# The upper part of SBUF of a fused attention and mixer kernel begins 224 bytes lower

## The chip, the cores and the metric

The kernel runs on one core of one Trainium2 chip. The metric is the device time of one execution in microseconds. All matrix products are float32-accurate: most operands are split into a high and a low part (type fp32r) and three products are added.

## The reference

Attention over 4 batches of 12 heads (sequence 448, head size 64, capped scores) gives x of (4, 448, 768). Two mixer layers follow:

```python
scores = cap * np.tanh(scale * q @ k.T / cap)         # scale = 1/8
x = softmax(scores) @ v                               # heads side by side: (4, 448, 768)

theta = x @ w_theta                                   # 768 x 768
y = w_tok_r @ (x * cos(theta)) + w_tok_i @ (x * sin(theta))   # 448 x 448 each, over tokens
u = x + y
x = u + relu(u @ w_ch)                                # 768 x 768

h = relu(x.T @ w_tok1) @ w_tok2                       # 448 -> 256 -> 448, over tokens
u = x + h.T
out = u + relu(u @ w_ch1) @ w_ch2                     # 768 -> 1536 -> 768, the MLP
```

## The kernel before, in words

**Stages.** TensorE works through five stages, each written out as a fixed order of instructions with semaphore waits. The times are those of the profiled execution.

- Attention, to about 179 us: 24 pairs of heads. `score` makes scores 448 columns wide with two 64-row matmuls side by side, `weigh_slot` and `sum_keys` multiply by values and by ones.
- Angles and token mixing, 179 to 388 us, by batch: `angles(b)` multiplies x (x_hi, x_lo as weights) by theta (moving, 384 columns), and `mix_tokens(b, half)` multiplies z (weights) by the token matrices (moving, 448 columns).
- Channel and token layers, 388 to 551 us, by batch: `channel(b, e)` has channel_hi, channel_lo as weights and u as the moving operand, 448 columns, in sets of 18 matmuls. `turn` transposes. `tokens_up` has tok1 as weights and 384 columns moving, in sets of 24. `tokens_down` has hidden as weights and tok2 as the moving operand, 448 columns, six matmuls for each feature tile; three of those in a row are 18 matmuls.
- MLP, 547 us to the end: four blocks of tokens k = 0 to 3 (512, 384, 512, 384 wide). For each of the twelve weight tiles c, `up(k, c)` does 18 matmuls with wide as the moving operand and `down(k, c)` does 18 with relu. The order is up 0, up 1, down 0, up 2, down 1, and so on to up 11, down 10, down 11. Every one of them reads its weights from tile mlp[c] and moves 512 or 384 columns.

`products` (L1047 to L1051) issues the three matmuls of one split product: hi by hi (L1049), hi by lo (L1050), lo by hi (L1051). In the program matmul(out, weights, moving), the trace prints the moving operand and the weights of a matmul in no fixed order.

**Placement.** SBUF addresses are written out by hand, as byte offsets within a partition. BASE is 16512 = 64.5 x 256. The constants lie from there; x_t begins at 17664 = 69 x 256; the working memory AT_WORK (L63) at 60672 = 237 x 256, and the upper memory AT_TOP (L64) at 167392 = 653 x 256 + 224. Every tensor in the working and the upper memory lies a multiple of 256 bytes behind the start of its region. In the working memory are x_hi and x_lo, z, u, wide, rows, hidden, and the MLP's tiles 0, 1 and 7 to 10, with one relu buffer; tile 11 and two relu buffers lie in the second half of x_t. In the upper memory lie, one after another in time:

- theta_hi, theta_lo, token_hi, token_lo (L142 to L145), moving operands;
- channel_hi, channel_lo and their raw copy (L187 to L190), tok1_hi, tok1_lo (L191, L192), weights, and tok2_hi, tok2_lo (L193, L194), moving operands;
- the MLP's tiles 2 to 6, weights, by

```python
tile_at = ([AT_EARLY + 12288 * j for j in range(2)] + [AT_TOP + 12288 * j for j in range(5)]
           + [AT_ROWS + 12288 * j for j in range(4)] + [AT_X + X_BYTES // 2])
```

Within a tile, one matmul's weights are 128 elements of 4 bytes, at multiples of 512 bytes.

**Other engines.** The DMA queue of SyncE loads raw weights into place (L482, L485 for the MLP's tiles, as soon as the memory is free). GpSimd (`split`, L537 to L542), ScalarE (L755) and VectorE (L1027) split them into hi and lo in place. ScalarE and VectorE also take results out of PSUM.

Of the kernel before, what the change touches and what calls it, by code (L numbers as in the profile page):

```python
# [58 lines left out]
BASE = 16512  # L59
# [1 line left out]
AT_X = AT_SMALL + 1152  # L61
X_BYTES = BATCH * D_TILES * SEQ * 4
AT_WORK = AT_X + X_BYTES  # L63
AT_TOP = BASE + 150848 + 32  # L64


def mixer_kernel(nc, kq_t, v, cap, w_theta, w_tok_r_t, w_tok_i_t, w_ch, w_tok1, w_tok2,
                 w_ch1, w_ch2, out_t, sum_scratch, inverse_scratch, u_scratch):
    ctx = ExitStack()
    with ctx:  # L70
        def place(name, shape, dtype, offset):
            return nc.alloc_sbuf_tensor_at(name, shape, dtype, offset=offset)
# [65 lines left out]
        o += 2 * SUM_F * 4  # L138
        assert o <= AT_TOP


        theta_hi = place("theta_hi", [P, D_TILES, MODEL], F32R, AT_TOP)  # L142
        theta_lo = place("theta_lo", [P, D_TILES, MODEL], F32R, AT_TOP + 18432)
        token_hi = place("token_hi", [P, MIX_TILES, SEQ], F32R, AT_TOP + 36864)
        token_lo = place("token_lo", [P, MIX_TILES, SEQ], F32R, AT_TOP + 49408)  # L145
        o = AT_WORK
# [36 lines left out]
        turns = [turns0, place("turns1", [P, HALF], F32, o)]  # L183
        assert o + 1536 <= AT_TOP

# [1187 lines left out]
```

## Time and profile before

| what | value |
| --- | --- |
| median of 3 runs | 907.78 us (905.97 to 907.85) |
| profiled execution | 907.67 us |
| its span, first to last instruction | 905.6 us |
| TensorE busy, matmuls | 888.3 us, 5248 instructions |
| VectorE, ScalarE, GpSimd busy | 438.0, 305.4, 189.0 us |
| mean granted TensorE clock | 0.995 |

The page gives busy time and counts; the timeline gives each instruction with its start. In the timeline a matmul's duration includes its way through the array, so successive matmuls overlap: the distance from start to start, called the pitch here, is what a matmul costs. A pitch over a long run is the difference between two starts, divided by the number of matmuls between them, which the loops give.

### The profile page before, as it was taken

The page shows a single profiled execution, that of the slowest core. Times are in us where ns is not written, and L with a number is a line of the kernel's source. Part 1 is how long each engine was busy: PE and PEld are TensorE (multiplying, and loading weights), DVE is VectorE, ACT ScalarE, POOL GpSimd, SP SyncE. Part 2 cuts the span into 40 slices and gives each one's busy share as a digit, 9 for nine tenths or more (in the row PEclk, how much of TensorE's full clock was granted, in tenths as well). Part 3 has the DMA queues.
Part 4 walks back from the last instruction along what each step waited for, and adds up shares of the span by engine and source line. Part 5 has one row for each costly group of instructions (what it writes and reads, how often), then busy time and mean ns, then how long its engine had stood idle before and what let it go on. Part 6 is the DMA issues. An engine that isn't in the chain of part 4 may idle for free.

```text
span 905.6 us, 12431 instructions
## 1 busy us (share of the span) xinstructions
PE 888.3 (98%) x5248; PEld 746.3 (82%) x5248; DVE 438.0 (48%) x593; ACT 305.4 (34%) x355; POOL 189.0 (21%) x139
## 2 busy tenths in 40 slices
PE   8999999998999999999999999999999999999998
PEld 5455544498999889999999998888899988889998
DVE  5799988889484976824342433311400130003002
ACT  6989997644151433502121221111100100001000
POOL 0345535147050442451000005800000000000000
PEclk9999999999999999999999999999999999999999
DMA  7555674412020100330000115500220030002001
GB/s 175 160 133 146 176 175 115 124 43 62 1 70 1 39 23 1 106 111 1 1 0 1 62 47 187 176 1 1 70 71 1 1 105 0 1 1 71 1 1 53
DMA packets 42119, 56.84 MB, mean 63 GB/s; under 512 B 7344, under 2 KB 37456, under 8 KB 42064
## 3 DMA queue, kind: packets, MB, share of 16 engines
q1 hardware_dynamic: 41840, 55.82, 21.3%
q8 instruction: 42, 0.69, 0.3%
q10 hardware_dynamic: 224, 0.23, 0.1%
q14 instruction: 13, 0.11, 0.0%
HBM read 41.62 MB, written 8.52 MB: 55 GB/s over the span
## 4 chain that ended last, share of the span: by engine, by line
PE 88%; DVE 7%; issue 2%; ACT 1%; DMA 0%; POOL 0%; DVEq 0%; ACTq 0%
PE psum L1049 23%; PE psum L1050 23%; PE psum L1051 23%; PE psum L1091 8%; PE psum L1061 5%; PE psum L1066 2%; PE psum L1118 2%; DVE sin_z L899 1%; PE psum L1214 1%; DVE reduced L892 1%; DVE reduced L888 1%; DVE wide_lo L936 1%; ACT wide_hi L697 1%; PE psum L1164 1%; DMA kq_raw<-kq_t 0%
## 5 line engine op out<-in xcount | busy, mean ns | idle before, releaser
L1032 DVE SCALAR_TENSOR_TENSOR relu_lo<-psum,relu_hi 128x512 fp32r<-128x512 f32 (+1 forms) x48 | 30.0, 624 | 275.1 <-ACT relu_hi L761 217.3
L761 ACT ACTIVATE relu_hi<-psum 128x512 fp32r<-128x512 f32 (+1 forms) x48 | 26.2, 545 | 307.8 <-PE psum L1051 298.1
L1049 PE MATMUL psum<-wide_hi,mlp 128*128 128x512 f32 (+1 forms) x288 | 105.0, 365 | 0.4 <-DVE wide_lo L936 0.4
L1051 PE MATMUL psum<-wide_hi,mlp 128*128 128x512 f32 (+1 forms) x288 | 104.9, 364 | 0.0
L1051 PE MATMUL psum<-relu_hi,mlp 128*128 128x512 f32 (+1 forms) x288 | 104.8, 364 | 0.0
L1049 PE MATMUL psum<-relu_hi,mlp 128*128 128x512 f32 (+1 forms) x288 | 104.8, 364 | 0.0
L1050 PE MATMUL psum<-wide_lo,mlp 128*128 128x512 f32 (+1 forms) x288 | 104.8, 364 | 0.0
L1050 PE MATMUL psum<-relu_lo,mlp 128*128 128x512 f32 (+1 forms) x288 | 104.7, 364 | 0.0
L1091 PE MATMUL psum<-ring,values 128*32 128x448 f32 x768 | 81.4, 542 | 1.4 <-issue 1.2
L633 ACT ACTIVATE ring<-psum,score_scale 128x1792 f32<-128x1792 f32 (+1 forms) x48 | 75.2, 1566 | 18.8 <-PE psum L1118 10.3
L636 ACT ACTIVATE ring<-ring,cap_col 128x1792 f32<-128x1792 f32 (+1 forms) x48 | 77.1, 1606 | 1.6
L1049 PEld LDWEIGHTS psum<-wide_hi,mlp 128*128 128x128 f32 x288 | 54.0, 188 | 7.0 <-DVE wide_lo L936 1.1
L1091 PEld LDWEIGHTS psum<-ring,values 128*32 128x32 f32 x768 | 23.0, 109 | 44.5 <-issue 44.2
L1050 PEld LDWEIGHTS psum<-relu_lo,mlp 128*128 128x128 f32 x288 | 54.1, 188 | 6.1
L1051 PEld LDWEIGHTS psum<-wide_hi,mlp 128*128 128x128 f32 x288 | 54.0, 188 | 6.1
L1051 PEld LDWEIGHTS psum<-relu_hi,mlp 128*128 128x128 f32 x288 | 54.1, 188 | 6.1
L1050 PEld LDWEIGHTS psum<-wide_lo,mlp 128*128 128x128 f32 x288 | 54.0, 188 | 6.1
L1049 PEld LDWEIGHTS psum<-relu_hi,mlp 128*128 128x128 f32 x288 | 54.0, 188 | 6.0
L1049 PE MATMUL psum<-theta_hi,x_hi 128*128 128x384 f32 x168 | 58.7, 349 | 0.0
L1050 PE MATMUL psum<-theta_lo,x_hi 128*128 128x384 f32 x168 | 56.5, 336 | 0.0
L1051 PE MATMUL psum<-theta_hi,x_lo 128*128 128x384 f32 x168 | 56.5, 336 | 0.0
L1049 PE MATMUL psum<-u_hi,channel_hi 128*128 128x448 f32 x144 | 54.1, 375 | 0.0
(135 smaller groups left out, 1977.2 us busy)
## 6 DMA issues: line engine op xcount, KB each, us to landing
kq_raw<-kq_t SPq DMA_DIRECT2D x47, 224.0 KB, 3.8
mlp_raw<-moe_w_ch SPq DMA_DIRECT2D x24, 384.0 KB, 6.8
values<-v SPq DMA_DIRECT2D x48, 112.0 KB, 3.3
inverse_rows<-inverse_scratch SPq DMA_DIRECT2D x12, 448.0 KB, 6.0
x_batch<-x_t SPq DMA_DIRECT2D x4, 1344.0 KB, 6.4
u_scratch<-x_t SPq DMA_DIRECT2D x2, 1344.0 KB, 5.6
out_t<-x_t SPq DMA_DIRECT2D x4, 672.0 KB, 3.4
theta_raw<-moe_w_theta SPq DMA_DIRECT2D x6, 384.0 KB, 4.5
```

The source lines that it names most:

```text
L633: act.activation(places, psum[:, first:end, 0:SEQ], ACT.Tanh, scale=score_scale[:, :]).then_inc(tanh_done, 1)
L636: act.activation(places, places, ACT.Exp, scale=cap_col[:, :]).then_inc(probs_ready, 1)
L697: act.activation(wide_hi[:, :, 0:BLOCKS[k][1] - BLOCKS[k][0]], x_block(k), ACT.Copy).then_inc(u_hi_made, 1)
L761: act.activation(relu_hi[c % 3][:, 0:n_tokens], psum[:, c % 2, 0:n_tokens], ACT.Relu).then_inc(relu_hi_made, 1)
L1032: dve.scalar_tensor_tensor(out=relu_lo[c % 3][:, 0:n_tokens], in0=psum[:, c % 2, 0:n_tokens], scalar=0.0, in1=relu_hi[c % 3][:, 0:n_tokens ...
L1049: pe.matmul(out, left[0], right[0], start=start, stop=False)
L1050: pe.matmul(out, left[0], right[1], start=False, stop=False)
L1051: return pe.matmul(out, left[1], right[0], start=False, stop=stop)
L1061: b_mm = pe.matmul(psum[:, b_tile, 0:SEQ], left[s][b_rows, b_keys], right[s][b_rows, queries], start=step == 0, stop=step == 2 and b_tile ...
L1066: a_mm = pe.matmul(psum[:, a_tile, 0:SEQ], left[s][a_rows, a_keys], right[s][a_rows, queries], start=step == 0 and a_tile != T, stop=step ...
L1091: mm = pe.matmul(psum[rows, VALUES_BANK, 0:SEQ], own[:, block, 32 * h:32 * h + 32], ring[:, ring_place(pair, tile), :], start=n == 0, stop ...
L1118: mm = pe.matmul(psum[32 * n:32 * n + 32, SUMS_BANK, 0:SEQ], weights[:, :], moving, start=True, stop=True)
```

## The change

One constant is changed. The upper memory begins at BASE + 150656 = 167168 = 653 x 256, where it began at BASE + 150880 = 167392. Everything placed relative to AT_TOP moves down by 224 bytes. The last tensor below it (sums) ends at 167104. No instruction, wait or size changes.

```diff
--- before.py
+++ after.py
@@ -61,7 +61,7 @@
 AT_X = AT_SMALL + 1152
 X_BYTES = BATCH * D_TILES * SEQ * 4
 AT_WORK = AT_X + X_BYTES
-AT_TOP = BASE + 150848 + 32
+AT_TOP = BASE + 150656
 
 
 def mixer_kernel(nc, kq_t, v, cap, w_theta, w_tok_r_t, w_tok_i_t, w_ch, w_tok1, w_tok2,
```

## Rows read from the trace of the kernel before

**Rows 1.** The page: busy time by engine; shares of the chain that ended last.
```profile
PE 888.3 (98%) x5248; PEld 746.3 (82%) x5248; DVE 438.0 (48%) x593; ACT 305.4 (34%) x355; POOL 189.0 (21%) x139
...
PE 88%; DVE 7%; issue 2%; ACT 1%; DMA 0%; POOL 0%; DVEq 0%; ACTq 0%
```
**Rows 2.** Stretches: length, busy PE, PEld, DVE, ACT, POOL, clock, DMA share, GB/s.
```profile
213.00:262.00 49.00, 49.00 (x263) 46.43 (x262) 35.41 (x56) 17.52 (x34) 16.61 (x14) 0.99 0.11 32
...
300.00:330.00 30.00, 27.77 (x151) 25.94 (x150) 28.77 (x45) 14.84 (x31) 15.60 (x14) 1.00 0.16 47
...
392.00:548.00 156.00, 155.95 (x831) 144.83 (x830) 63.09 (x88) 31.90 (x44) 21.80 (x14) 1.00 0.11 37
548.00:650.00 102.00, 102.00 (x448) 83.64 (x447) 27.36 (x33) 16.54 (x24) 26.43 (x19) 1.00 0.21 68
```
**Rows 3.** TensorE's waits, the longest: us in total, times, longest us.
```profile
PE psum L1049 <- DVE sin_z L899: 4.8, 2, 2.5
```
**Rows 4.** Timeline of TensorE, MLP block 0: start us, length us, instruction.
```profile
571.95 0.39 PE L1049 MATMUL psum<-wide_hi,mlp 128*128 128x512 f32 x1
...
605.54 0.39 PE L1049 MATMUL psum<-wide_hi,mlp 128*128 128x512 f32 x1
...
622.02 0.39 PE L1049 MATMUL psum<-wide_hi,mlp 128*128 128x512 f32 x1
...
646.50 0.39 PE L1049 MATMUL psum<-relu_hi,mlp 128*128 128x512 f32 x1
```
**Rows 5.** The same view, MLP block 1.
```profile
666.27 0.34 PE L1049 MATMUL psum<-wide_hi,mlp 128*128 128x384 f32 x1
...
691.71 0.33 PE L1049 MATMUL psum<-wide_hi,mlp 128*128 128x384 f32 x1
...
704.26 0.33 PE L1049 MATMUL psum<-wide_hi,mlp 128*128 128x384 f32 x1
...
722.98 0.33 PE L1049 MATMUL psum<-relu_hi,mlp 128*128 128x384 f32 x1
```
**Rows 6.** The same view: tokens_up, channel, tokens_down of batch 0.
```profile
421.02 0.34 PE L1049 MATMUL psum<-rows_hi,tok_hi 112*128 112x384 f32 x1
...
425.26 0.37 PE L1049 MATMUL psum<-u_hi,channel_hi 128*128 128x448 f32 x1
...
428.97 0.36 PE L1049 MATMUL psum<-tok_hi,hidden_hi 128*128 128x448 f32 x1
...
429.57 0.37 PE L1049 MATMUL psum<-tok_hi,hidden_hi 128*128 128x448 f32 x1
...
432.64 0.36 PE L1049 MATMUL psum<-u_hi,channel_hi 128*128 128x448 f32 x1
```
**Rows 7.** The same view: scores of pairs 8 and 9 of heads.
```profile
61.09 0.36 PE L1066 MATMUL psum<-kq_hi,kq_lo 64*128 64x448 f32 x1
...
62.33 0.36 PE L1066 MATMUL psum<-kq_hi,kq_lo 64*128 64x448 f32 x1
...
67.76 0.36 PE L1061 MATMUL psum<-kq_lo,kq_hi 64*128 64x448 f32 x1
...
69.18 0.36 PE L1061 MATMUL psum<-kq_hi,kq_lo 64*128 64x448 f32 x1
```
**Rows 8.** The same view: token mixing of batch 1, then angles of batch 2.
```profile
259.19 0.45 PE L1049 MATMUL psum<-token_hi,tail_hi 128*128 128x448 f32 x1
...
284.90 0.34 PE L1049 MATMUL psum<-theta_hi,x_hi 128*128 128x384 f32 x1
...
288.03 0.27 PE L1164 MATMUL psum<-ident,x_batch 128*128 128x128 f32 x1
```
**Rows 9.** Splits of the MLP's tiles, duration min/median/max in ns; timeline of GpSimd.
```profile
L539 POOL CAST mlp<-mlp_raw x14: 823/826/1435, 400.5 to 582.7; 128x768 fp32r<-128x768 f32 x14
...
L1027 DVE TENSOR_TENSOR mlp<-mlp_raw,mlp x10: 958/959/2345, 563.6 to 635.8; 128x768 fp32r<-128x768 f32 x10
...
543.29 0.82 POOL L539 CAST mlp<-mlp_raw 128x768 fp32r<-128x768 f32 x1 [131.60 <-DMA mlp_raw<-moe_w_ch]
```

## The prediction

> **What bounds the kernel now.** I read the page first: TensorE is busy 98% of the span and the chain that ended last is 88% TensorE [rows 1]. Then I read the table of stretches. It shows TensorE busy 49.00 of 49.00 us busy in the stretch of 213 to 262 us, 155.95 of 156.00 us in the channel and token stretch, and 102.00 of 102.00 us in the first MLP block, at a granted clock of 0.99 to 1.00, the upper of its two levels (2.4 GHz) [rows 2]. The table of TensorE's waits has nine rows and 13 us in all, none of it for a DMA; the longest is 4.8 us in two waits for the angles [rows 3]. A busy share of 100% doesn't say that the engine streams at its best pace, since a matmul's record (0.39 us) is longer than the distance between two starts (0.23 us). So the view that decides here is the timeline of TensorE, read as pitch: start of one matmul to the start of the next. Any pitch that shrinks moves the end almost one for one.
>
> **The natural experiment in the trace.** The MLP uses twelve weight tiles of one shape in one loop, up(c) and down(c-1) by turns, 18 matmuls each. Tiles 2 to 6 begin at AT_TOP + 12288 j. AT_TOP is 167392 = 653 x 256 + 224, which is 32 beyond a multiple of 64; all other tiles, and the moving operands wide and relu, begin on multiples of 256. For 512 columns, from the start of up(0,3) at 571.95 to that of up(0,7) at 605.54 lie eight phases, 144 matmuls, that all read tiles 2 to 6: 33.59 / 144 = 233.3 ns. From up(0,9) at 622.02 to down(0,11) at 646.50 lie six phases, 108 matmuls, of tiles 8 to 11: 24.48 / 108 = 226.7 ns [rows 4]. For 384 columns the same two stretches are 25.44 / 144 = 176.7 ns and 18.72 / 108 = 173.3 ns [rows 5]. Instruction, clock, moving operand and neighbours are the same; the place of the weights is what differs. So weights in the upper memory cost 6.6 ns per matmul of 512 columns and 3.4 ns per one of 384.
>
> **The change, part by part.** It adds and removes no instruction and no wait. It moves everything that is placed from AT_TOP down by 224 bytes, to 653 x 256.
>
> *MLP.* Five tiles x 36 matmuls x two blocks of 512 columns: 360 x 6.6 = 2.4 us. The two blocks of 384: 360 x 3.4 = 1.2 us. Together 3.6 us, all on the path.
>
> *tok1 weights.* 192 matmuls of 384 columns take their weights there. One set of 24 runs from 421.02 to 425.26: 176.7 ns [rows 6], the slow pace of 384. At the good one: 192 x 3.4 = 0.65 us.
>
> *Channel weights.* 432 matmuls of 448 columns. The set of 18 that follows runs from 425.26 to 428.97, 206.1 ns [rows 6]. No row shows an ordinary 448-column matmul of all 128 rows with both operands on a multiple of 64, so I bound it. Lower bound: the line through the two good paces, 173.3 at 384 and 226.7 at 512, gives 200.0 at 448, a gain of 432 x 6.1 = 2.6 us. Upper bound: the scores are 448 columns wide and have both operands on multiples of 256; pair 8 of heads runs at 1.24 us for six steps, 206.7 ns, so the gain may be 0. Pair 9 runs at 1.42 us for seven, 202.9 ns [rows 7]. The token mixing (weights low, moving operand high) has 25.71 / 126 = 204.0 ns with its first gap in it [rows 8], and a set of tok2 3.67 / 18 = 203.9 [rows 6]. Three of four rows lie near 203.3, so I take that: 432 x 2.8 = 1.2 us.
>
> *Upper memory as the moving operand.* theta (504 matmuls, 384 columns): from 284.90 to 288.03, 3.13 / 18 = 173.9 ns [rows 8], the good pace but for 0.6, so between nothing and 0.3 us is to be had; I take nothing. token and tok2 (648 matmuls, 448 columns): between 200.0 (a gain of 648 x 4 = 2.6 us) and the 206.7 of pair 8 (a loss of 1.8 us). theta says that a moving operand off the boundary costs nothing, and pair 9 that 203 is what 448 columns do on aligned operands, so I take 203.5 and 0.3 us.
>
> *Writers and transfers.* GpSimd, ScalarE and VectorE split weights in either memory. For the MLP's tiles, on and off the boundary mixed, the shortest and the middle duration are 823 and 826 ns on GpSimd, 958 and 959 on VectorE [rows 9]; the move is worth nothing to them. The loads into the upper memory may take a little less or more: GpSimd waits for the tiles' data, but TensorE waits for none of that [rows 3]. Tile 2's data are there at 543.29 [rows 9], and TensorE comes to it two phases of 4.2 us before the 571.95 of [rows 4], at about 563.6. With some 6 us for the split in between, a landing would have to slip by over 10 us to cost anything. Where the matmuls get faster, nothing else is late: in the MLP stretches VectorE is busy 27 of 102 us and ScalarE 17 [rows 2]. Only around the angles do the chains of VectorE and GpSimd set the pace (2.2 us idle in the stretch from 300 to 330, and the 4.8 us above) [rows 2, 3], and the move doesn't touch those.
>
> **A rule against it.** The Trainium skill, "SBUF — State Buffer", section Specifications (TRN2), gives SBUF 16-byte cachelines and names no wider grid for speed. Both 167392 and 167168 are multiples of 16, so by that rule the move does nothing and the time stays at 907.7 us, as in the fourth rival below. The rows disagree with it as the whole story: 233.3 against 226.7 ns between operands that all begin on multiples of 16. The same page, Operand start alignment, treats a start as a matter of legality and says it timed nothing.
>
> **The sum.** The profiled execution took 907.67 us (span 905.6, 2.05 around it), 0.1 under the median of 907.78. 3.6 + 0.65 + 1.2 + 0.3 = 5.75, so 907.7 - 5.8 = 901.9 us, 0.63% less.
>
> **The rivals.**
> First, everything goes to the floor: misplacement, of either operand, is all that 448 columns suffer from. Then 3.6 + 0.65 + 2.6 + 2.6 = 9.45, 898.3 us. For it: the first three matmuls of a tok2 set take 0.60 us, 200 ns each [rows 6]. Against: pairs 8 and 9, aligned and at 207 and 203; theta, off the boundary and free.
> Second, the 448-column streams keep what they have or fall into the slow rhythm of pair 8: only 4.25 us of the MLP and tok1 remain (903.4), or 4.25 - 1.8 = 2.45 us (905.2). For it: the channel's 206.1 is nearly pair 8's pace with everything aligned.
> Third, slower: what marks tiles 2 to 6 is that they lie high, not their residue, and the move brings moving operands onto the residue of their weights (x_hi and theta, z and token, hidden and tok2 differ by 224 now). If equal residues collide, 648 matmuls go from 204.0 to 206.7 (+1.8 us) and theta's 504 from 173.3 to 176.7 (+1.7): 911.2 us. It ends slower only if the MLP's and tok1's 4.25 us stay out, since they would outweigh its 3.5. Against: MLP tiles 7 to 11 share their residue with wide and relu and are the fast ones.
> Fourth, the change doesn't do what it says: the border is one of place. The highest fast tile ends at 158976 and the lowest slow one begins at 167392, so no row excludes a border between them. Then nothing moves, 907.7. Against: tok1's, channel's and the five tiles' weights, spread over 60 KB, all lose alike, while theta, in the same place, loses nothing as a moving operand.
>
> **How the numbers follow.** Forecast (901.0 to 903.0) 0.48; all to the floor 0.22; 448 columns unchanged or slow 0.17; place alone 0.09; slower 0.04. A measurement of this kernel can tell about 0.2% (1.8 us) from no change. Faster are the first three, 0.87; the same 0.09; slower 0.04. For 8 in 10 the range takes the forecast, the floor and the milder half of the third case (903.4 but not 905.2), with 0.8 us of scatter at the low end and 1.0 at the high one: 897.5 to 904.4.
>
> **What would show it.** In the profile of the changed kernel the eight phases from up(0,3) to up(0,7) should take 144 x 226.7 = 32.6 us in place of 33.6, and the 384-column ones 25.0 in place of 25.4; tok1's sets 4.16 in place of 4.24. The channel's 18 matmuls at 3.60 us speak for the floor, 3.66 for the forecast, 3.71 for the second rival; the token stretch of 126 at 25.2 us for the floor, 25.7 for the forecast. Stages before 179 us should not change. I am wrong if the upper tiles keep 233.3 ns, or if another operand, theta above all, takes up a pitch over 173.3.

## The result, and the profile after

The changed kernel takes 903.82 us (median of 13 runs, 900.37 to 906.29) against 907.85 us (13 runs, 905.45 to 910.65). The ratio is 0.9949, 95% interval 0.9933 to 0.9966: 4.6 us less (3.1 to 6.1), which is the distance of the two means; the medians are 4.0 apart. A good part of the scatter goes with the granted TensorE clock: of the changed kernel's 13 executions the one at a mean of 0.998 took 900.37 us and the one at 0.992 took 906.29. The forecast was 901.9 us and 5.8 us less, with a range of 897.5 to 904.4.

The profiled execution took 904.51 us, its span is 902.5. The page's line of busy times answers to [rows 1]; TensorE is still busy 98% of it.
```profile
PE 885.0 (98%) x5248; PEld 745.9 (83%) x5248; DVE 436.8 (48%) x593; ACT 305.7 (34%) x355; POOL 188.5 (21%) x139
```
The timeline of TensorE after, in the MLP's blocks 0 and 1 (start us, length us, instruction). From up(0,3) to up(0,7), and from up(1,3) to up(1,7), as in [rows 4, 5]:
```profile
572.45 0.39 PE L1049 MATMUL psum<-wide_hi,mlp 128*128 128x512 f32 x1
...
605.09 0.39 PE L1049 MATMUL psum<-wide_hi,mlp 128*128 128x512 f32 x1
...
665.60 0.33 PE L1049 MATMUL psum<-wide_hi,mlp 128*128 128x384 f32 x1
...
690.55 0.33 PE L1049 MATMUL psum<-wide_hi,mlp 128*128 128x384 f32 x1
```
32.64 / 144 = 226.7 ns where it was 233.3, and 24.95 / 144 = 173.3 where it was 176.7. All twelve tiles now have the good pace.

The 448-column stages after, same view: the channel's first two sets of batch 0, then a tok1 set and the channel set behind it (to answer to [rows 6]), then the token mixing of batches 1 and 3, whose ends are 285.45 and the 389.07 above (to answer to [rows 8]).
```profile
389.07 0.37 PE L1049 MATMUL psum<-u_hi,channel_hi 128*128 128x448 f32 x1
...
396.51 0.27 PE L1214 MATMUL psum<-ident,block_t 128*112 128x128 f32 x1
...
421.74 0.34 PE L1049 MATMUL psum<-rows_hi,tok_hi 112*128 112x384 f32 x1
...
425.93 0.36 PE L1049 MATMUL psum<-u_hi,channel_hi 128*128 128x448 f32 x1
...
429.58 0.36 PE L1049 MATMUL psum<-tok_hi,hidden_hi 128*128 128x448 f32 x1
```
```profile
259.83 0.45 PE L1049 MATMUL psum<-token_hi,tail_hi 128*128 128x448 f32 x1
...
285.45 0.34 PE L1049 MATMUL psum<-theta_hi,x_hi 128*128 128x384 f32 x1
...
362.96 0.45 PE L1049 MATMUL psum<-token_hi,tail_hi 128*128 128x448 f32 x1
```
The channel knows two rhythms: 7.44 / 36 = 206.7 ns in the first sets and 3.65 / 18 = 202.8 in most later ones (steady 206.7 in five of the 24 sets and 202.7 in nineteen; all 24 had 206.7 before). Token mixing has 25.62 / 126 = 203.3 in batch 1, but 26.11 / 126 = 207.2 in batch 3, which was 25.85 / 126 = 205.2 before:
```profile
362.39 0.45 PE L1049 MATMUL psum<-token_hi,tail_hi 128*128 128x448 f32 x1
...
388.24 0.36 PE L1049 MATMUL psum<-u_hi,channel_hi 128*128 128x448 f32 x1
```
A wait has grown. TensorE's waits for wide_lo (us in total, times, longest), first before, then after:
```profile
PE psum L1049 <- DVE wide_lo L936: 0.4, 1, 0.4
...
PE psum L1049 <- DVE wide_lo L936: 1.9, 2, 1.6
```
The timelines of GpSimd and VectorE there, first after, then before:
```profile
543.16 1.84 POOL L541 TENSOR_TENSOR mlp<-mlp_raw,mlp 128x768 fp32r<-128x768 f32 x1
...
543.42 4.79 DVE L936 TENSOR_TENSOR wide_lo<-x_t,wide_hi 128x3072 fp32r<-128x3072 f32 x1 [1.45 <-ACT wide_hi L697]
```
```profile
544.12 3.36 DVE L936 TENSOR_TENSOR wide_lo<-x_t,wide_hi 128x3072 fp32r<-128x3072 f32 x1 [1.44 <-ACT wide_hi L697]
...
544.20 4.97 POOL L541 TENSOR_TENSOR mlp<-mlp_raw,mlp 128x768 fp32r<-128x768 f32 x1
```
Before, VectorE began 0.08 us ahead of GpSimd: its subtraction took 3.36 us and GpSimd's took 4.97 in place of 1.84. After, tile 2's data had landed a little earlier, GpSimd began 0.26 us ahead, and VectorE's took 4.79. TensorE stood for 1.6 us before up(0,0), where it had stood 0.4; from the last tok1 matmul to up(0,0) it is 1.89 us in place of 0.39, 1.5 more.

Where the time went, by stage, from the starts on the timeline (us):

| stage | before | after |
| --- | --- | --- |
| attention, to the first theta matmul | 178.86 | 179.44 |
| angles and token mixing | 209.38 | 209.63 |
| channel and token layers, to the first MLP matmul | 159.29 | 159.20 |
| MLP, to the end | 358.10 | 354.24 |
| from the angles to the end | 726.77 | 723.07 |

The last row is the one to compare between single profiles: in the profiles of this study the attention stage ended anywhere from 175.79 to 182.25 us, although no kernel changes anything that TensorE, ScalarE or VectorE read there. Part of that is the clock: from 12 to 22 us the granted clock was 0.66 after and 1.00 before. By groups of matmuls (sums of pitches) the 3.7 us are: MLP -2.6 at 512 columns and -1.2 at 384, channel -1.1, tok1 -0.4, tok2 -0.2, theta -0.1, token +0.4, and the wait for wide_lo +1.5.

### The profile page after: what moved, and what is told of

Same layout as the page of the kernel before. It is cut to its first block, busy times and chain, and to the rows that moved or that the text cites. A ratio compares the mean times of both kernels' runs of the same rounds, so it can differ in the third digit from the quotient of the medians.

```text
span 902.5 us, 12431 instructions
## 1 busy us (share of the span) xinstructions
PE 885.0 (98%) x5248; PEld 745.9 (83%) x5248; DVE 436.8 (48%) x593; ACT 305.7 (34%) x355; POOL 188.5 (21%) x139
## 4 chain that ended last, share of the span: by engine, by line
PE 89%; DVE 6%; issue 2%; ACT 1%; POOL 0%; DVEq 0%; POOLq 0%; ACTq 0%
PE psum L1049 23%; PE psum L1051 23%; PE psum L1050 23%; PE psum L1091 9%; PE psum L1061 5%; PE psum L1066 3%; PE psum L1118 2%; DVE sin_z L899 1%; PE psum L1214 1%; DVE wide_lo L936 1%; DVE reduced L892 1%; DVE reduced L888 1%; PE psum L1124 1%; ACT wide_hi L697 1%; PE psum L1164 1%
## 5 line engine op out<-in xcount | busy, mean ns | idle before, releaser
L1049 PE MATMUL psum<-token_hi,z_hi 128*128 128x448 f32 x144 | 53.4, 371 | 0.5 <-POOL z_lo L592 0.5
```

What stands on the lines that cost most here:

```text
L1049: pe.matmul(out, left[0], right[0], start=start, stop=False)
```

## Experiments

The theory of the prediction was that weights must begin on a boundary. Its rivals were the place (high memory), and, new after the result, the distance between the start of the weights and that of the moving operand. "Distance" is weights minus moving operand, modulo 256.

**The lower tiles off the boundary, the upper ones on it.**
```diff
-        tile_at = ([AT_EARLY + 12288 * j for j in range(2)] + [AT_TOP + 12288 * j for j in range(5)]
-                   + [AT_ROWS + 12288 * j for j in range(4)] + [AT_X + X_BYTES // 2])
+        tile_at = ([AT_EARLY + 32 + 12288 * j for j in range(2)] + [AT_TOP + 12288 * j for j in range(5)]
+                   + [AT_ROWS + 32 + 12288 * j for j in range(4)] + [AT_X + X_BYTES // 2])
-        ring_at = [o, AT_X ...
+        ring_at = [o + 256, AT_X ...
```


> The changed kernel, but the MLP's six tiles in the lower memory (0, 1, 7 to 10) begin 32 bytes past a multiple of 256, and the five in the upper memory stay on it. Theory of the residue: every phase of tiles 0, 1, 7 to 10 takes the slow pace (233.3 ns a matmul at 512 columns, 176.7 at 384; 4.20 and 3.18 us a phase), tiles 2 to 6 and 11 the good one (226.7 and 173.4). That is 6 x 36 x 2 x (6.6 + 3.4) = 4.3 us more than the changed kernel, about 908. Rival of the place (what counts is that weights lie above 160 KB): all tiles keep the pace of the changed kernel, about 904.

One execution: 909.74 us (the kernel before, same chip, 908.51). Its timeline: up(0,3) to up(0,7) on upper tiles; up(0,9) to up(0,11), four phases on tiles 8 to 10; the same four at 384 columns.
```profile
575.05 0.39 PE L1049 MATMUL psum<-wide_hi,mlp 128*128 128x512 f32 x1
...
607.70 0.39 PE L1049 MATMUL psum<-wide_hi,mlp 128*128 128x512 f32 x1
...
624.38 0.40 PE L1049 MATMUL psum<-wide_hi,mlp 128*128 128x512 f32 x1
...
641.18 0.39 PE L1049 MATMUL psum<-wide_hi,mlp 128*128 128x512 f32 x1
...
706.68 0.34 PE L1049 MATMUL psum<-wide_hi,mlp 128*128 128x384 f32 x1
...
719.17 0.35 PE L1049 MATMUL psum<-wide_hi,mlp 128*128 128x384 f32 x1
```
Upper tiles 32.65 / 144 = 226.7 ns, lower ones 16.80 / 72 = 233.3. The roles have changed places, so the rival of the place falls. But at 384 columns the lower tiles have 12.49 / 72 = 173.5, not the expected 176.7: weights 32 beyond the boundary are free there, weights at 224 were not. The whole MLP stage takes 358.88 us, 4.6 more than the changed kernel's, which looks like the 4.3 of the theory but is chance: the six tiles cost 432 x 6.6 = 2.9 us at 512 columns and next to nothing at 384, and 1.65 us are in up(0,0) (5.85 us for 18 matmuls, 4.20 at 233.3 ns). There eight matmuls started 427 ns apart, at a granted clock of 0.50 from 550 to 553 us, the lower of the two levels (1.2 GHz), after TensorE had stood 1.8 us for wide_lo.

**A residue for each tile.** Tiles shifted by (160, 192, 0, 32, 64, 96, 224, 32, 64, 96, 128, 0) bytes, tok1 and tok2 moved on by 256 to make room.

> The changed kernel with each MLP tile at a residue of its own, modulo 256: tiles 0 to 11 at 160, 192, 0, 32, 64, 96, 224, 32, 64, 96, 128, 0. If a multiple of 64 is what weights need, tiles 1, 2, 4, 8, 10 and 11 have 226.7 ns and tiles 0, 3, 5, 6, 7, 9 (odd multiples of 32) have 233.3. If it is 256, as in the words of the change, only tiles 2 and 11 are fast; if it is 128, tiles 2, 10 and 11. The residue modulo 256 may also give more than two paces.

908.03 us in one execution. Two of its phases at 512 columns, up(0,1) (residue 192) and up(0,10) (residue 128):
```profile
554.02 0.39 PE L1051 MATMUL psum<-wide_hi,mlp 128*128 128x512 f32 x1
...
558.15 0.39 PE L1051 MATMUL psum<-relu_hi,mlp 128*128 128x512 f32 x1
...
629.30 0.39 PE L1051 MATMUL psum<-wide_hi,mlp 128*128 128x512 f32 x1
...
633.49 0.39 PE L1051 MATMUL psum<-relu_hi,mlp 128*128 128x512 f32 x1
```
4.13 and 4.19 us, against 4.08 at the good pace. The steady pitches (the second half of each phase, from the starts, ns; a range is over up and down and the tiles of that residue):

| residue | 0 | 32 | 64 | 96 | 128 | 160 | 192 | 224 |
| --- | --- | --- | --- | --- | --- | --- | --- | --- |
| 512 columns | 226.7 | 233.2-233.6 | 233.3-233.7 | 233.9-235.0 | 232.2-233.3 | 233.3 | 228.9 | 233.0-233.3 |
| 384 columns | 173.3 | 173.3 | 174.3-176.8 | 173.3-176.4 | 175.3-176.1 | 176.7-177.1 | 173.3 | 173.3-176.4 |

Multiples of 64 or 128 don't do. Of eight residues only 0 has the good pace at both widths. At 384 columns one residue can have either pace (224: 173.3 in up, 176.4 in down), so something besides the residue plays a part there, perhaps the tile read just before.

**The moving operands off, the weights on.** wide and relu, high and low, begin 32 bytes on; what lies behind wide moves by 256.
```diff
-        wide_hi = place("wide_hi", [P, D_TILES, BANK], F32R, o)
-        wide_lo = place("wide_lo", [P, D_TILES, BANK], F32R, o + 12288)
-        o += 24576
+        wide_hi = place("wide_hi", [P, D_TILES, BANK], F32R, o + 32)
+        wide_lo = place("wide_lo", [P, D_TILES, BANK], F32R, o + 12288 + 32)
+        o += 24576 + 256
```


> The changed kernel, all weights on multiples of 256, but the MLP's moving operands (wide and relu, high and low parts) begin 32 bytes past one. Theory (only the start of the weights counts, as theta seemed to say): pitches stay at 226.7 and 173.4 ns. Rival (the distance between the two starts counts): 233.3 and 176.7 everywhere, 1728 x 5 = 8.6 us more than the changed kernel.

912.34 us in one execution. The same four starts as at the top:
```profile
572.46 0.39 PE L1049 MATMUL psum<-wide_hi,mlp 128*128 128x512 f32 x1
...
606.06 0.39 PE L1049 MATMUL psum<-wide_hi,mlp 128*128 128x512 f32 x1
...
668.16 0.34 PE L1049 MATMUL psum<-wide_hi,mlp 128*128 128x384 f32 x1
...
693.60 0.34 PE L1049 MATMUL psum<-wide_hi,mlp 128*128 128x384 f32 x1
```
33.60 / 144 = 233.3 and 25.44 / 144 = 176.7 ns, with all weights on multiples of 256, and so in every tile but for the first phase. The MLP takes 362.68 us where the changed kernel takes 354.24: 8.4 more, 8.6 were the rival's. The theory that only the start of the weights counts is refuted. The distance is 0 - 32 = -32 here, and it was 224 - 0 = -32 in [rows 4, 5]: the same two pitches.

**Both off.** Every tensor from the channel on, weights and moving operands alike, 32 bytes on (AT_TOP + 32, AT_WORK + 32 for u and what follows, tile 11 and the relu buffers + 32).

> The changed kernel with weights and moving operands of all stages after the token mixing 32 bytes past a multiple of 256, so that both have one residue. Theory (the start of the weights by itself): 233.3 and 176.7 ns in all twelve MLP tiles, 8.6 us more than the changed kernel, and 206 to 207 in the channel. Rival (their distance): 226.7 and 173.4 everywhere.

898.80 us in one execution; 721.01 us from the angles to the end. Its timeline: up(0,3) to up(0,7); a theta set; the token mixing of batch 1.
```profile
566.75 0.39 PE L1049 MATMUL psum<-wide_hi,mlp 128*128 128x512 f32 x1
...
599.39 0.39 PE L1049 MATMUL psum<-wide_hi,mlp 128*128 128x512 f32 x1
```
```profile
235.23 0.34 PE L1049 MATMUL psum<-theta_hi,x_hi 128*128 128x384 f32 x1
...
238.41 0.27 PE L1164 MATMUL psum<-ident,x_batch 128*128 128x128 f32 x1
...
256.07 0.45 PE L1049 MATMUL psum<-token_hi,tail_hi 128*128 128x448 f32 x1
...
281.36 0.33 PE L1049 MATMUL psum<-theta_hi,x_hi 128*128 128x384 f32 x1
```
32.64 / 144 = 226.7 ns with not one operand of the MLP on a multiple of 64. It is the distance of the two starts, not either start. theta tests its sign: its distance, x_hi minus theta, was 0 - 224 = +32 before and is 0 - 32 = -32 here. This set has 3.18 / 18 = 176.7 ns, the pace of distance -32 at 384 columns, which 11 of this run's 28 theta sets have; the other 17 have a steady 173.4. And the token stretch has 25.29 / 126 = 200.7 with its first gap in it, a steady 200.0, the floor that the prediction had worked out (e9 comes back to it).

**Distance 256.** The upper tiles, tok1 and tok2 are 256 bytes further on, on even multiples of 256, with the moving operands on odd ones.

> The changed kernel with the MLP's upper tiles (2 to 6) and tok1, tok2 256 bytes further on, so that they lie on even multiples of 256 while the moving operands stay on odd ones. If a distance of a multiple of 256 is what counts, tiles 2 to 6 keep 226.7 and 173.4 ns and the channel its 202.7 to 206.7. If it must be a multiple of 512, tiles 2 to 6 have more (229 to 233 ns at 512 columns).

904.72 us in one execution.
```profile
572.69 0.39 PE L1049 MATMUL psum<-wide_hi,mlp 128*128 128x512 f32 x1
...
605.33 0.39 PE L1049 MATMUL psum<-wide_hi,mlp 128*128 128x512 f32 x1
```
32.64 / 144 = 226.7: a distance of 256 is as good as 0. The grid of 256 bytes is right, for the distance.

**One part of the change: the weights alone.** theta, token and tok2 keep residue 224 (their offsets + 224), channel, tok1 and the tiles are as changed.

> One part of the change: channel, tok1 and the MLP's upper tiles are on a multiple of 256 as in the changed kernel, while theta, token and tok2, which are moving operands, keep residue 224. By my sum of the change this holds 5.45 of its 5.75 us, the rest being token and tok2. From the trace of the changed kernel I now expect slightly more: the token stretches had 204.0 to 204.5 ns before and 202.9 or 206.7 after, 0.4 us more in all, so this kernel should be level with the changed one within 0.5 us, and its token stretches at the pitches of before.

903.84 us (12 runs), ratio to the kernel before 0.9961 (0.9944 to 0.9977). From the angles to the end it takes 722.81 us against 723.07, and its token stretches have the steady pitches of before (203.3 in batch 1, 204.4 in batch 3). The gain of the change is that of the weights, as forecast.

**GpSimd waits for wide_lo.** In the loop over the MLP's tiles, on the changed kernel, and on the kernel before:
```diff
             for c in range(C_TILES):
+                if c == 2:
+                    pool.wait_ge(u_lo_made, BATCH + 1)
                 pool.wait_ge(mlp_loaded[c], 32)
```


> The changed kernel, and GpSimd waits for wide_lo of block 0 before it splits the MLP's tile 2. Theory: in the changed kernel's trace VectorE's wide_lo took 4.79 us where it took 3.36 before, because GpSimd's subtraction began 0.26 us ahead of it and held it up; TensorE stood 1.6 us before up(0,0). With the wait wide_lo takes 3.3 to 3.4 us, TensorE's wait for it falls to about 0.4 us, and the time falls by 1.2 us against the changed kernel (about 902.6). Rival (wide_lo's length is from something else, or TensorE is held by ScalarE's wide_hi): no change.

902.45 us (6 runs), ratio to the kernel before 0.9947 (0.9930 to 0.9964), where the changed kernel's is 0.9949: the times don't separate the two. The trace does (VectorE's and GpSimd's timelines, TensorE's wait; the two added lines shift the line numbers by 2):
```profile
544.58 3.36 DVE L938 TENSOR_TENSOR wide_lo<-x_t,wide_hi 128x3072 fp32r<-128x3072 f32 x1 [1.44 <-ACT wide_hi L699]
```
```profile
PE psum L1051 <- DVE wide_lo L938: 0.4, 1, 0.4
```
The channel and token stage takes 157.45 us against 159.20. So the collision is real. It costs 1.4 us (0.46 us from the last tok1 matmul to up(0,0), in place of 1.89) where 1.2 were expected. The other 0.3 of the 1.75 are not its doing: none of the channel's 24 sets has the slow rhythm here, and five had it in the changed kernel. Elsewhere this execution was slower: 26.12 us for batch 1's token mixing, the slow rhythm, in place of 25.62, and 27.66 for batch 2's in place of 26.64, with a granted clock of 0.72 from 316 to 322 us where the changed kernel had 1.00 (315 to 321). So from the angles to the end there is only 0.5 us between them. What follows matters for every reading at 448 columns: the two kernels give TensorE the same instructions and addresses, and yet batch 1's tokens run at a steady 202.7 ns in one profile and at 206.7 in the other.

> The kernel before with the same wait of GpSimd as in the run before. In its profiled execution wide_lo had won the race (3.36 us, TensorE waited 0.4 us). If it always wins there, no change (within 0.3 us); if the race goes either way from one execution to the next, up to 0.6 us faster on the median.

907.73 us (12 runs), ratio 1.0011 (0.9999 to 1.0023): no gain, and the stage takes 159.29 us, to the hundredth what it took without the wait. The race, without the wait, in the profiles: won by VectorE before and in e2, e3 and e4, lost after and in e1, e5, e7 and e10. In these profiles VectorE began wide_lo 5.39 to 5.40 us after the first issue of tile 2's loads, and GpSimd its first pass over the tile, 0.9 us ahead of its subtraction, 4.57 us after it before and, with tile 2 at the one address of the changed kernel, anywhere from 4.23 to 4.51. The order turns at about 4.49. That the move itself makes the data come earlier is not shown: there is one such profile of the kernel before.

**The pitch by number of columns.** All operands on multiples of 256, rows of the moving operand 2048 bytes apart.
```diff
-                tokens = slice(0, BLOCKS[k][1] - BLOCKS[k][0])
+                tokens = slice(0, min(COLUMNS.get(k, [BANK] * C_TILES)[c], BLOCKS[k][1] - BLOCKS[k][0]))
```


> The changed kernel, but up and down of MLP blocks 0 and 2 move fewer columns, so part of the products is left out. Columns by tile 0 to 11: block 0 has 512, 512, 480, 464, 448, 432, 416, 400, 384, 368, 352, 336; block 2 has 512, 512, 488, 472, 456, 440, 424, 408, 392, 320, 288, 256. Both operands lie on multiples of 256 and rows are 2048 bytes apart. If 448 columns as such don't stream at the floor, the phases at 448 show 203 or 207 ns and neighbours that floor = columns/2.4 + 13.3 ns (480: 213.3, 416: 186.7) or not, by their number. If it was the row distance of 1792 bytes in the channel that hurt, 448 columns have 200.0 here.

The phases with 448 columns (up(0,4)), 480 (up(0,2)) and 400 (up(0,7)), each with the first matmul of the next:
```profile
577.96 0.36 PE L1049 MATMUL psum<-wide_hi,mlp 128*128 128x448 f32 x1
...
581.60 0.37 PE L1049 MATMUL psum<-relu_hi,mlp 128*128 128x464 f32 x1
```
```profile
562.29 0.38 PE L1049 MATMUL psum<-wide_hi,mlp 128*128 128x480 f32 x1
...
566.20 0.39 PE L1049 MATMUL psum<-relu_hi,mlp 128*128 128x512 f32 x1
...
599.44 0.34 PE L1049 MATMUL psum<-wide_hi,mlp 128*128 128x400 f32 x1
...
602.68 0.35 PE L1049 MATMUL psum<-relu_hi,mlp 128*128 128x416 f32 x1
```
3.64 / 18 = 202.2 ns, 217.2 and 180.0. The steady pitches of the up phases, beside the floor, columns / 2.4 + 13.3, which is the line through the two good paces:

| columns | 512 | 480 | 464 | 448 | 440 | 432 | 416 | 408 | 400 | 392 | 384 | 352 | 336 | 320 | 288 | 256 |
| --- | --- | --- | --- | --- | --- | --- | --- | --- | --- | --- | --- | --- | --- | --- | --- | --- |
| floor ns | 226.6 | 213.3 | 206.6 | 200.0 | 196.6 | 193.3 | 186.6 | 183.3 | 180.0 | 176.6 | 173.3 | 160.0 | 153.3 | 146.6 | 133.3 | 120.0 |
| measured | 226.7 | 216.2 | 209.4 | 202.8 | 200.0 | 196.0 | 188.7 | 184.9 | 180.0 | 177.3 | 173.3 | 160.9 | 153.3 | 146.7 | 131.4 | 120.0 |

448 columns miss the floor by 2.8 ns with both operands aligned and rows 2048 bytes apart; the row distance of 1792 isn't the cause. From 408 to 488 columns (488: 224.8 for 216.6) none reaches it, and 392 and 352 miss it by less than 1 ns. And it is no floor in the strict sense: 288 columns run 1.9 ns below it.

**Token matrices at distance -32.** The one stretch at 200.0 ns, tried for itself, with GpSimd's wait.
```diff
-        token_hi = place("token_hi", [P, MIX_TILES, SEQ], F32R, AT_TOP + 36864)
-        token_lo = place("token_lo", [P, MIX_TILES, SEQ], F32R, AT_TOP + 49408)
+        token_hi = place("token_hi", [P, MIX_TILES, SEQ], F32R, AT_TOP + 36864 + 32)
+        token_lo = place("token_lo", [P, MIX_TILES, SEQ], F32R, AT_TOP + 49408 + 32)
```


> The changed kernel with GpSimd's wait of run e6, and token_hi and token_lo 32 bytes past a multiple of 256 while z, their weights, lies on one. This is the distance -32 (weights minus moving operand) of the run with everything off, where the token stretch of batch 1 had 200.0 ns a matmul at 448 columns. Theory (the distance decides): the token stretches have 204.5 and 200.0 ns for batches 0 and 1 as there, against 206.7 and 202.7 in the changed kernel, and the MLP keeps 226.7 and 173.4. From the start of the angles to the end: 721.0 to 721.5 us, 1.2 to 1.5 less than e6's 722.55; median 901 to 902. Rival (what quickened that stretch was something else): pitches of 202.7 and 206.7, and 722.5 us.

902.09 us (6 runs), ratio 0.9935 (0.9911 to 0.9958), which doesn't separate it from e6's; 721.66 us from the angles to the end. The token stretches have a steady 206.7 ns in batches 0, 1 and 3: the expectation on the pitch missed. But batch 2, before the wait in its middle and behind it, has the 200.0 again:
```profile
318.63 0.36 PE L1051 MATMUL psum<-token_hi,z_hi 128*128 128x448 f32 x1
...
325.83 0.36 PE L1051 MATMUL psum<-token_hi,z_hi 128*128 128x448 f32 x1
```
7.20 / 36 = 200.0. The steady paces of the token stretches in all twelve profiles sort by distance: 203.3 and 204.4 ns at +32 (before, e5, e8), 202.7 and 206.7 at 0 (after, e1, e2, e3, e6, e7, e10), 200.0, 204.4 and 206.7 at -32 (e4 and here). So in these profiles the distance goes with the rhythms that occur, and doesn't say which of them a stretch takes; the changed kernel and e6 have the same placement and differ in batch 1. What chooses is open; it may be the moment at which the stretch begins.

## Why the prediction was right, and where not

**Read as pitch.** That TensorE's starts, not its busy share, show the cost, and that each nanosecond of pitch moves the end, held: the MLP stage fell by 3.86 us.

**MLP, 3.6 us.** Measured 3.8. The pitches came to 226.7 and 173.3 ns as put down. Most of the 0.2 more are the phases of tiles 1 and 8, which no longer need a few matmuls to settle behind a slow tile.

**The mechanism.** Here a step failed without harm to the sum, and that was luck: after the change every operand of the MLP, the channel and tok1 begins on a multiple of 256, where "weights on the boundary" and "distance 0" say the same. "theta says that a moving operand off the boundary costs nothing" was the wrong reading of [rows 8]: theta lay at distance +32, which is free at 384 columns (173.5 ns in e1, with the weights off); at distance -32 the same theta has 176.7 in 11 of 28 sets of e4. Moving operands count as much as weights (e3: +8.4 us), and the kernel with everything off loses nothing (e4). The change helps because it brings the upper weights to distance 0 from wide, relu, u and rows. The reason given against the third rival, that tiles sharing a residue with wide are the fast ones, was this rule; I had it in hand and didn't draw it.

**The rivals.** Place alone is refuted by e1, equal residues as a loss by e4. The Trainium skill's 16-byte lines ("SBUF — State Buffer", Specifications (TRN2)) don't describe this cost: all starts are multiples of 32, and pitches still range from 226.7 to 235.0 ns (e2).

**tok1, 0.65 us.** Measured 0.4. The steady pitch is 173.3, but each set of 24 begins with some seven matmuls that settle (4.19 us, not 4.16).

**Channel, 1.2 us.** Measured 1.1. The value from pair 9's row, 203, was right, and pair 8's row too: 19 sets have the one rhythm, five the other (in e6, with the same placement, none has the slow one, so 1.1 is the value of this profile). 202.8 ns is what 448 columns take on aligned operands (e7). Neither the floor nor the second rival came true, though the five slow sets are the second rival in small.

**token and tok2, 0.3 us.** Measured +0.2: tok2 gave 0.2, the token stretches lost 0.4, since batches 0 and 3 fell into 206.7. It lay inside the bounds named, -2.6 to +1.8, and its sign is that of this profile: in e3, e7 and e10 batch 0 has 202.7, 0.4 us less.

**The step that failed: "the writers and transfers are worth nothing".** I asked how late a landing may be and found 10 us. I didn't ask what an earlier one does. SyncE's first issue of tile 2's loads and GpSimd's first pass over its data after, and the issue before (the pass before is at 543.29, [rows 9]):
```profile
538.03 0.37 SPq L482 DMA_DIRECT2D mlp_raw<-moe_w_ch  x1
...
542.26 0.82 POOL L539 CAST mlp<-mlp_raw 128x768 fp32r<-128x768 f32 x1 [129.75 <-DMA mlp_raw<-moe_w_ch]
```
```profile
538.72 0.37 SPq L482 DMA_DIRECT2D mlp_raw<-moe_w_ch  x1
```
The data came 4.23 us after the issue in place of 4.57, GpSimd's subtraction began before VectorE's wide_lo, and TensorE lost 1.5 us. The trace before had the signs of it: GpSimd's 4.97 us beside its usual 1.84 at 544.20, and wide_lo beginning 0.08 us before it. Take 1.5 us for that and 0.9 for tok1, channel, token and tok2 from the 5.75 of the sum, add 0.3 for MLP and theta, and the 3.7 of the profile is there. The median of the runs gives 4.6 with an interval that holds both 3.7 and 5.75; how often the race is lost over many executions isn't known (of the eight profiles with the upper memory moved and no wait, five lost it), and the wait put on the changed kernel could not be told from none by its time.

## What to carry to other kernels

Look for a natural experiment in the trace before asking what a layout is worth: the same instruction on tensors in different places, read as the distance between starts over a hundred matmuls. Then move each operand by itself and both together, because one pair of places fits more than one rule. Place the weights and the moving operand of an fp32r matmul a multiple of 256 bytes apart (shown here at 512 and 384 columns); it is the distance that has to be kept, not the boundary itself. And where two engines begin within a tenth of a microsecond of each other and one then takes more than twice its usual time, the order can go either way: price it both ways, for things that come earlier too.

## What the runs showed of the hardware

- The pitch of fp32r matmuls depends on the distance of the two starts modulo 256: at 512 columns 226.7 ns at 0, about 233.3 at most others, 228.9 at 192.
- The sign counts at 384 columns: 173.4 at +32 everywhere (e1, theta before), but at -32 176.7 in the MLP before and in e3, and in e2's down phase and 11 of e4's 28 theta sets about the same, while e2's up phase and the other 17 sets had 173.4.
- Widths from 408 to 488 columns don't reach columns / 2.4 + 13.3 ns even at distance 0, while 400, 384, 336, 320 and 256 do, and 288 lies 1.9 ns below it (e7).
- Streams of 448 columns mostly hold one rhythm for a whole stretch (200.0, 202.7, 203.3, 204.4 or 206.7 ns) and change it only at a break; with the same placement it can differ from one execution to the next (after and e6). The scores do so too: pair 8 had 206.7 ns and pair 9 202.9 before [rows 7], and after the change, which touches nothing of theirs, pair 8 has 202.9 and pair 9 206.7.
- A GpSimd subtraction and a VectorE subtraction in SBUF don't share: whichever began first ran at its own time (1.84 or 3.36 us) and the other was longer (4.79 or 4.97 us) by what was left of the first, less 0.15 us.
